# Router keys, choices and digits of three batches computed inside the attention loop, with 68 empty steps ahead of the VectorE program

## The reference

```
attention, per batch b (4), head h (8), step t (768), head size 64:
  state = gamma[h] * state + outer(k[t], v[t])
  y[t]  = (1/8) * q[t] @ state
x = y laid out as 3072 tokens x 512

mixture of experts, 8 experts, 384 tokens each:
  logits = x @ w_gate                       (3072 x 8)
  all 24576 logits, largest first: a token not yet assigned goes to
  the expert of that logit, if the expert has fewer than 384 tokens
  out[tokens of e] = relu(x @ w1[e]) @ w2[e]

gated unit:  (sigmoid(x @ w_gate2) * (x @ w_val)) @ w_out
```

## Time and profile before

| | us |
|---|---|
| three executions | 1081.01, 1081.10, 1082.03 |
| the profiled execution's own time | 1080.85 |
| its span, first to last instruction | 1079.1 |
| PE matmul busy | 1026.2 (95%) |
| PE weight load busy | 956.1 (89%) |
| DVE busy | 701.6 (65%) |
| ACT busy | 326.6 (30%) |
| POOL busy | 123.4 (11%) |

### The profile page before, as it was taken

How to read it: one execution, slowest core, us unless ns; L and a number is a source line. 1 busy time by engine, 2 the same in 40 slices (tenths; PEclk the granted TensorE clock), 3 DMA queues, 4 the chain that set the end, 5 groups by cost and what they waited for, 6 DMA issues and landing times.

```text
span 1079.1 us, 20068 instructions
## 1 busy us (share of the span) xinstructions
PE 1026.2 (95%) x7130; PEld 956.1 (89%) x7130; DVE 701.6 (65%) x1880; ACT 326.6 (30%) x622; POOL 123.4 (11%) x149
## 2 busy tenths in 40 slices
PE   8999726999999999999999999999999999999996
PEld 7888616899999999999999999999999999999995
DVE  4877777787577657765776677667775677554211
ACT  3222144322342233323332233223422341234210
POOL 4423203243000101010101010001001100110001
PEclk9999956999999999999999999999999999999998
DMA  8999564304141324132412332143214231423000
GB/s 201 221 220 239 138 196 147 98 20 127 52 136 39 88 79 134 53 88 78 128 60 69 97 109 79 50 118 99 88 39 128 81 107 39 124 73 117 1 1 30
DMA packets 197356, 107.69 MB, mean 100 GB/s; under 512 B 81936, under 2 KB 182800, under 8 KB 197264
## 3 DMA queue, kind: packets, MB, share of 16 engines
q1 hardware_dynamic: 193424, 93.94, 31.5%
q0 software_dynamic: 3840, 12.59, 3.7%
HBM read 88.41 MB, written 18.09 MB: 99 GB/s over the span
## 4 chain that ended last, share of the span: by engine, by line
PE 93%; DVE 3%; DMA 1%; issue 1%; SPq 1%; POOL 0%; ACT 0%; DVEq 0%; POOLq 0%
PE bank L1373 21%; PE bank L1375 21%; PE bank L1374 21%; PE bank L1466 6%; PE bank L1467 6%; PE bank L1465 6%; PE bank L659 2%; PE bank L729 2%; PE bank L725 2%; PE bank L1327 1%; PE bank L685 1%; PE bank L692 1%; PE bank L739 1%; PE bank L706 1%; PE bank L674 1%
## 5 line engine op out<-in xcount | busy, mean ns | idle before, releaser
L1373 PE MATMUL bank<-h2h,resident 128*128 128x384 f32 x768 | 261.2, 340 | 0.0
L1375 PE MATMUL bank<-h2h,resident 128*128 128x384 f32 x768 | 257.9, 336 | 0.0
L1374 PE MATMUL bank<-h2l,resident 128*128 128x384 f32 x768 | 257.3, 335 | 0.0
L1373 PEld LDWEIGHTS bank<-h2h,resident 128*128 128x128 f32 x768 | 144.3, 188 | 2.9
L1374 PEld LDWEIGHTS bank<-h2l,resident 128*128 128x128 f32 x768 | 144.3, 188 | 2.9
L1375 PEld LDWEIGHTS bank<-h2h,resident 128*128 128x128 f32 x768 | 144.1, 188 | 0.0
L883 ACT ACTIVATE ring<-ring_raw 128x512 fp32r<-128x512 f32 x192 | 117.6, 623 | 54.6 <-DMA ring_raw<-in_moe_w_out_dram 41.8
L1200 DVE TENSOR_TENSOR pf<-bank,gate 128x384 f32<-128x384 f32 x96 | 53.5, 557 | 121.0 <-PE bank L1375 113.2
L1209 DVE TENSOR_TENSOR ring<-ring_raw,ring 128x512 fp32r<-128x512 f32 x192 | 127.3, 689 | 0.0
L907 ACT ACTIVATE ph<-pf 128x384 fp32r<-128x384 f32 x96 | 50.4, 525 | 252.4 <-DVE pf L1200 252.4
L1204 DVE TENSOR_TENSOR pl<-pf,ph 128x384 fp32r<-128x384 f32 x96 | 54.2, 564 | 56.8 <-ACT ph L907 56.8
(11 more groups left out here) (193 smaller groups left out, 1648.5 us busy)
## 6 DMA issues: line engine op xcount, KB each, us to landing
ring_raw<-in_moe_w_dram SPq DMA_DIRECT2D x128, 256.0 KB, 3.1
ring_raw<-in_moe_w_out_dram SPq DMA_DIRECT2D x64, 256.0 KB, 2.9
qraw<-in_q_dram SPq DMA_DIRECT2D x24, 256.0 KB, 3.5
kraw<-in_k_dram SPq DMA_DIRECT2D x24, 256.0 KB, 4.2
vraw<-in_v_dram SPq DMA_DIRECT2D x24, 256.0 KB, 4.2
xrows<-xrow SPq DMA_DIRECT2D x96, 64.0 KB, 2.1
xlaid<-xg SPq DMA_DIRECT2D x7, 768.0 KB, 4.4
zg<-xlaid SPq DMA_DIRECT2D x28, 192.0 KB, 4.2
```

Of the source, the lines that this page charges most:

```text
L1373: nc.tensor.matmul(ps, wh, xhi, start=start, stop=False)
L1374: nc.tensor.matmul(ps, wh, xlo, start=False, stop=False)
L1375: return nc.tensor.matmul(ps, wl, xhi, start=False, stop=stop)
```

## The change

In slots c = 4 and c = 5 of each turn of the attention loop (b = 1, 2, 3), after `mask_scores`, DVE now also runs `prepare_ahead(b, 0)` and `prepare_ahead(b, 1)`: the keys, then the choice and the digits, of the six tiles of batch b - 1. After the attention only the last batch's six tiles are done (`prepare_last`), with the product by `unassigned` (L1044) left out of it. The operations are the same as in the old preparation, on 6 tiles in place of 24 (48 elements a partition in place of 192, 6 in place of 24, 42 in place of 168). The steps of `dve_chain` in the preparation go from 13 to 45. Ahead of everything that waits, DVE's program gets 68 instructions that only add 1 to a semaphore that nobody waits for. The preparation for the later experts is as it was.

```diff
--- before.py
+++ after.py
@@ -53,13 +53,14 @@
         DIGITS = -(-32 // RADIX_BITS)
         NEG = -3.4028234663852886e38
         BIG = 1.0e6
-        PREP_CHAIN = 13
         FIRST_CHAIN = 79
         ROUTE_CHAIN = 125
-        CHAIN_START = PREP_CHAIN
+        UNIT_CHAIN = 11
+        CHAIN_START = (U // C) * UNIT_CHAIN + 1
         TABLES = 8 + 5 + 3 + 3
 
         RING = 8
+        VECTOR_LEAD = 68
         STREAMED = KF + 2 * KD + RING
         OUT_STREAMED = STREAMED - KF - 2 * KD
         RESIDENT = 3 * KG - OUT_STREAMED
@@ -325,6 +326,7 @@
             k_loaded = [sem(f"k_loaded{c}") for c in range(C)]
             v_loaded = [sem(f"v_loaded{c}") for c in range(C)]
             state_cleared = sem("state_cleared")
+            lead = sem("lead")
             growth_turned = sem("growth_turned")
             growth_even = sem("growth_even")
             growth_odd = sem("growth_odd")
@@ -538,8 +540,10 @@
 
                 slots(act, body, 0, U + 3)
 
-            def attend_vector(dve):
+            def attend_vector(dve, prepare_ahead):
                 nc.vector.memset(state[:, :, :, :], 0.0).then_inc(state_cleared, 1)
+                for n in range(VECTOR_LEAD):
+                    dve.sem_inc(lead, 1)
 
                 def scale_growth(c):
                     dve.wait_ge(growth_turned, c + 1)
@@ -623,6 +627,8 @@
                         mask_scores(b, c, s)
                     if s in (1, 3):
                         scale_growth(s + 2)
+                    if s is None and c >= C - 2:
+                        prepare_ahead(b, c - C + 2)
 
                 slots(dve, body, 0, U + 4)
 
@@ -944,8 +950,6 @@
 
         @block.vector
         def _(dve):
-            attend_vector(dve)
-
             link_count = [0]
             link_base = [0]
 
@@ -1021,9 +1025,55 @@
                         count_only(last)
                 link(last)
 
-            def prepare(first):
+            def first_keys(n):
+
+                tiles = bass.ds(n * C, C)
+                logged = masked[:, :, tiles]
+                link(nc.vector.reduce_max(best[:, tiles], over_experts(logged), AX_X))
+                count_only(nc.vector.tensor_scalar(bits[:, tiles], best[:, tiles], 0.0, None, ALU.add))
+                link(nc.vector.tensor_tensor(wide[:, :, tiles], logged, best[:, tiles].unsqueeze(1).to_broadcast([P, E, C]), ALU.is_equal))
+                count_only(nc.vector.tensor_scalar(key[:, tiles], bits[:, tiles].bitcast(I32), 31, -2147483648,
+                                                   ALU.arith_shift_right, ALU.bitwise_or))
+                link(nc.vector.tensor_tensor(wide[:, :, tiles], wide[:, :, tiles],
+                                             priority[:, :].unsqueeze(2).to_broadcast([P, E, C]), ALU.mult))
+                count_only(nc.vector.tensor_tensor(key[:, tiles], key[:, tiles], bits[:, tiles].bitcast(I32), ALU.bitwise_xor))
+
+            def first_digits(n):
+
+                tiles = bass.ds(n * C, C)
+                link(nc.vector.reduce_max(top[:, 0, tiles], over_experts(wide[:, :, tiles]), AX_X))
+                count_only(nc.vector.tensor_tensor(digit_i[:, :, tiles], key[:, tiles].unsqueeze(1).to_broadcast([P, DIGITS, C]),
+                                                   shift[:, :].unsqueeze(2).to_broadcast([P, DIGITS, C]), ALU.logical_shift_right))
+                link(nc.vector.tensor_tensor(choice[:, :, tiles], priority[:, :].unsqueeze(2).to_broadcast([P, E, C]),
+                                             top[:, 0, tiles].unsqueeze(1).to_broadcast([P, E, C]), ALU.is_equal))
+                link(nc.vector.tensor_scalar(digit_i[:, :, tiles], digit_i[:, :, tiles], RADIX - 1, None, ALU.bitwise_and))
+                link(nc.vector.tensor_scalar(digit_f[:, :, tiles], digit_i[:, :, tiles], 1.0, None, ALU.add))
+
+            def prepare_ahead(b, part):
+
+                link_base[0] = (b - 1) * UNIT_CHAIN
+                link_count[0] = 0 if part == 0 else 6
+                if part == 0:
+                    dve.wait_ge(tables_made, TABLES)
+                    dve.wait_ge(logits_saved, b * C)
+                    first_keys(b - 1)
+                    assert link_count[0] == 6
+                else:
+                    first_digits(b - 1)
+                    assert link_count[0] == UNIT_CHAIN
+
+            def prepare_last():
+
+                link_base[0] = 0
+                link_count[0] = (B - 1) * UNIT_CHAIN
+                first_keys(B - 1)
+                first_digits(B - 1)
+                compare_first(digit_f[:, 0, :])
+                raise_by(digit_f[:, 0, :], 1)
+
+            def prepare():
                 prepare_keys()
-                prepare_digits(first)
+                prepare_digits()
 
             def prepare_keys():
 
@@ -1036,7 +1086,7 @@
                 link(nc.vector.tensor_tensor(wide[:, :, :], wide[:, :, :], per_expert(priority[:, :]), ALU.mult))
                 count_only(nc.vector.tensor_tensor(key[:, :], key[:, :], bits[:, :].bitcast(I32), ALU.bitwise_xor))
 
-            def prepare_digits(first):
+            def prepare_digits():
 
                 link(nc.vector.reduce_max(top[:, 0, :], over_experts(wide[:, :, :]), AX_X))
                 count_only(nc.vector.tensor_tensor(digit_i[:, :, :], key[:, :].unsqueeze(1).to_broadcast([P, DIGITS, U]),
@@ -1045,10 +1095,7 @@
                 count_only(nc.vector.tensor_scalar(digit_i[:, :, :], digit_i[:, :, :], RADIX - 1, None, ALU.bitwise_and))
                 link(nc.vector.tensor_tensor(choice[:, :, :], per_expert(priority[:, :]), per_token(top[:, 1, :]), ALU.is_equal))
                 link(nc.vector.tensor_scalar(digit_f[:, :, :], digit_i[:, :, :], 1.0, None, ALU.add))
-                if first:
-                    compare_first(digit_f[:, 0, :])
-                else:
-                    compare(digit_f[:, 0, :])
+                compare(digit_f[:, 0, :])
                 raise_by(digit_f[:, 0, :], 1)
 
             def route(vis, i):
@@ -1243,7 +1290,7 @@
                         prepare_keys()
                         vis[0] += 1
                     elif vis[0] == VISITS + 2 and follows:
-                        prepare_digits(False)
+                        prepare_digits()
                         vis[0] += 1
 
                 if follows:
@@ -1282,11 +1329,11 @@
                     assert link_count[0] == ROUTE_CHAIN, link_count[0]
                 out_rows(i)
 
+            attend_vector(dve, prepare_ahead)
             dve.sem_inc(orow_ready, TT)
             dve.sem_inc(orow_free, 1)
-            dve.wait_ge(tables_made, TABLES)
             dve.wait_ge(logits_saved, U)
-            prepare(True)
+            prepare_last()
             assert link_count[0] == CHAIN_START, link_count[0]
             begin_route(0)
             for vis in range(VISITS):
@@ -1294,7 +1341,7 @@
             make_onehot(0)
             route_ids(0)
             close()
-            prepare(False)
+            prepare()
             assert link_count[0] == FIRST_CHAIN, link_count[0]
             for n in range(RING // 2):
                 piece_low(0, n)
```

## The result

| | us, median | lowest to highest | runs |
|---|---|---|---|
| before | 1080.53 | 1079.03 to 1082.12 | 19 |
| after | 1082.96 | 1079.68 to 1084.17 | 19 |

The ratio is 1.0019, its 95% interval 1.0012 to 1.0026: 2.05 us slower (1.3 to 2.8), just under the 2.16 us that I had set as the bound of no change. The two medians stand 2.43 us apart. The forecast was 1081.6 us, range 1079.2 to 1086.0. The profiled execution of after took 1083.55 us, span 1081.7, mean granted clock 0.976.

The account below looks back on a forecast made before the run. PE's work bounds the attention, DVE's chain the hole behind it. -1.54 + 1.5 + 0.5 + 0 = +0.46, say +0.5, on 1080.85 gives 1081.35; with 0.25 for the median, 1081.6 us, range 1079.2 to 1086.0.

Parts of the forecast that it names:

- What bounds the kernel: Attention: loop mask, y, xTa, state, mask is closed; an xTa delay is never regained. Behind it, DVE's chain sets the time.
- End of the preparation, -1.54: First maximum to first comparison after the attention: 2.10 us against 3.64, all on the path; bounds -1.2 and -1.8.
- Work in the slots, +1.5: Attention loop: five of 11 operations need a new address at once, 0.5 us a batch over three; bounds 0 and 6.1.
- POOL at the same time, +0.5: Attention slots: new DVE work meeting POOL's scaling of k loses up to 1.04 us each; half of one taken.
- The rival of POOL in step with both batches: Attention, first and second batch: three more meetings of 1 us beside the forecast, 1084.6 us; chance 0.08.
- Empty steps, 0: Program start: the 68 steps stand in DVE's idle time before the first mask and cost 0, at worst +0.5.
- Place of the code, no effect: Expert loop: longer DVE program moves its 1.59 us pause; gone, no gain; doubled without cover, 1092 us; growing-pause chance 0.03.

Follow-up runs that it names:

- POOL out of the way: The kernel after, with POOL scaling the first two k of batches 2 and 3 later; ratio 1.0007 (0.9998 to 1.0015) to the kernel before.
- the three edits together: The kernel after without empty steps, POOL's first two k of batches 2 and 3 later, last digit step only counted; 1079.48 us against 1080.21 for the kernel before.

## Why the prediction was right, and where it was off

**What bounds the kernel.** Right: PE's full attention is a closed loop with DVE, and a delay of xTa is paid, but for 0.21 us of a late digits' slot that came back in the next, which I had excluded. The sum from the slots and turns lies within 0.8 us of the ratio in all eleven rows of the table. What follows the comparison moved as a block within the 1.3 us by which it varies in all kernels.

**End of the preparation, -1.54.** Exact: 2.10 us in after, and 2.09 where the loop is written out (131.62 to 133.71).

**Work in the slots, +1.5.** The size holds, but by luck, for the mechanism was another. With POOL out of the way it was +1.84. I had put it on five address registers a batch, spread over both slots, and had no term for the loop's jump back. The keys' slots pay 0.01 to 0.38 us; the jump back behind the digits pays 0.5, with 0.2 more for the waited step, in two batches. I had assumed the three batches alike, and they are not: the third has no jump.

**POOL at the same time, +0.5.** This is the term that was mis-sized: 1.76 us in the profiled run (3.60 against 1.84), three meetings of some 0.6 us. I took half a meeting, reasoning from the slots of the second batch alone and writing "the first batch meets it little"; the first batch met it twice. One trace could not place that: in three kernels whose attention is that of before (before, empty steps alone, 12 steps alone) POOL begins this product 1.9, 3.0 and 3.2 us behind the xTa that opens the first batch's keys' slot, and the new keys stand at 2.7 to 4.1 us behind it. The rival of POOL in step with both batches, 1084.6 us, was the nearer picture of the mechanism, but its price of 1 us for each of three more meetings was too high. I also named only products with two inputs as exposed. The steps hit hardest have one (key<-bits, 0.81 and 0.85; the digit mask, 1.04 to 1.18). The Trainium skill (SBUF — State Buffer, section "SBUF: two separate sides") names as takers of the lock DVE operations with two inputs in SBUF and also those in a 2-port performance mode. The trace agrees that a step need not have two inputs to be hit; in which mode these steps ran, no row shows.

**Empty steps, 0.** Right: alone they leave every slot as it was and end in DVE's waits, and the ratio is 1.0000 (0.9990 to 1.0009). The difference of 0.5 us between the first two traces was not theirs.

**Place of the code, no effect.** Right for this change, and right too that PE gains nothing if the pause goes. But the rival was a real one and I gave it 0.03: 12 steps alone cost 4.2 us. The 68 steps leave the expert loop of this kernel as good as no steps do: the turns are 111.28 us with both. In the attention the keys' slots are 0.1 to 0.35 us longer with them at equal POOL (5.43, 5.20 and 5.20 against 5.08, 5.07 and 5.06), and in the first batch 0.29 us of idle time ends in no row. No packet of code begins near it (the next one 1.1 us behind it), so it isn't a pause like those of the expert loop, and its cause stays open.

Sum: forecast +0.46, measured +2.06 by the trace. The +1.6 between are POOL's 1.3 and the loop's 0.3. That the result still counts as no change is luck: 2.05 us against a bound of 2.16, inside an interval that reaches 2.8.

## What to carry to other kernels

Before work is moved into an engine's idle time, look at what the other engines run in that same time, here POOL's products, in every batch and in more than one trace: three meetings cost 1.76 us. In a loop keep waited work away from the jump back, or write the loop out. After any edit that changes an engine's number of instructions, read its idle time that ends in "issue", group by group: a shift of 12 instructions cost 4.2 us, twice what the whole change did.

## What the runs showed of the hardware

- The jump back of DVE's attention loop with its registers costs about 0.5 us when work stands right before it (digits' slots of 5.61 and 5.58 us with the three edits together), and nothing where the slot has 1.1 us of idle time (5.05 us in the kernel before).
- DVE's pause for code stood once in a turn of the expert loop (9.7 us in six turns), or twice (9.9 and 11.7 us), or not at all, by the offset of the loop alone.
- A step of 6 elements for each partition took up to 1.13 us beside a POOL product and 0.17 without one.
- Before the first growth DVE stood idle 5.62 us with 68 empty steps (5.63 in one of four kernels) and 6.83 us with 81. By these an empty step takes 0.08 to 0.09 us.
